# Attention and two MoE layers on one core: the order of exponentials, casts and low parts in the attention stage, and the first forget-gate rows spread by TensorE

## The chip, the cores and the metric

The kernel runs on one NeuronCore of one Trainium2 chip, in one launch. The metric is the device time of an execution in microseconds (us); a smaller one is better.

## The reference, cut to what matters

Attention with a forget gate over 4 batches, 8 heads, 576 positions and a head size of 64, then an MLP with a piecewise quadratic activation, then a top-1 mixture of 8 experts. What is computed ahead of the second layer:

```python
log_f = np.log(np.clip(f, 0.0001, 1.0))
cum = np.cumsum(log_f, axis=-1)
decay = cum[:, :, :, None] - cum[:, :, None, :]
scores = np.where(causal, -1000000000.0, scale * (q @ k.T) + decay)
scores = scores - np.max(scores, axis=-1, keepdims=True)
attn = np.exp(scores)
attn = attn / (np.sum(attn, axis=-1, keepdims=True) + 1e-09)
x = attn @ v            # heads merged to 2304 x 512
h = x @ w_in            # 512 -> 2048
g = np.where(h >= 1, h, np.where(h <= -1, 0.0, (h + 1) ** 2 / 4))
x = g @ w_out
# then: normalised x and expert_emb give logits / tau, one expert of 8 for each
# token, relu(x @ w1[e]) @ w2[e], times the gate
```

Along a row the term cum of the query is constant and drops out in the softmax, so the kernel only needs the row of the keys' cumulative sums, the same on all 64 query rows of a head.

## The kernel before, in words

All products that need more than one pass are made of a high part (rounded to the fp32r type) and a low part (what is left): high times high, high times low, low times high.

**Attention stage.** The 32 heads are 16 pairs; a pair has 9 query blocks of 64 rows. Both heads of a pair stand one above the other on the 128 partitions, so block i of a pair is a tile of 128 rows and 64(i+1) keys. The 144 tiles are steps n, with `tile_of(n)` giving the pair p and the block i. Each engine has one program written out by hand over n, and semaphores tie them together:

- TensorE (lines 1550 on, helpers at 1434 to 1510): `score(n + 4)` makes the scores of a tile in one of three PSUM banks and adds the causal mask (line 1431). The first two blocks of a pair are one f32 product (line 1447), the others three fp32r ones (1450, 1455). `turn(p, k)` (line 1477) transposes the weights of a pair in eight "fills", each a part of a PSUM bank; fill k needs the exponentials up to its block (0 after block 1, 1 after 3, 2 and 3 after 5, 4 and 5 after 7, 6 and 7 after 8), and as three banks are used in turn it waits for the low part of fill k-3, that is `pt_l`. Fill 7 also turns the inverse denominators of the pair before (1485). `head` (1494) multiplies with v. A score tile waits for the minimum three banks back (`minimum_ahead`): block 8 of a pair waits for the minimum of block 6.
- VectorE (lines 1172 to 1223): `masked(n)` (line 1112) reads the scores and the gate row `c8`, writes minus their scaled sum to `pr` and its minimum to `mmin`. `low(p, k)` (1134, 1131 for fill 7) subtracts the high part from the transposed weights. It also inverts denominators (1118, 1124), copies results (1140, 1146, 1150) and, in pairs 7 to 14, makes the low part of a tile of x (`split_x`, 1155). In step n it does `masked(n + 3)` and then the fills of step n-1.
- ScalarE (lines 902 to 923): `exp(n)` (864) is the exponential with its row sum; `high(p, k)` (874) casts a transposed fill to its high part; `copy_early` (880) copies a result. In step n it does `exp(n + 2)` and then the casts of the fills that belong to the block of step n-1; only where that block is 5 are the casts first:

```python
p, i = tile_of(n - 1)
if i != CASTS_FIRST and 0 <= n + 2 < STEPS:
    exp(n + 2)
if 0 <= n - 1 < STEPS:
    for k in fills_of(i):
        high(p, k)
if i == CASTS_FIRST and 0 <= n + 2 < STEPS:
    exp(n + 2)
```

- GpSimd splits k, q and v of later pairs into high and low parts (lines 624, 626, 638, 640, 648, 650) and adds and scales x (691, 693).
- SyncE issues the loads. The cumulative sums `fc`, which lie in the tile `pr`, are written to DRAM (line 470), and come back as a row broadcast over 64 partitions for each head (line 431; for the second head of pair 0 line 854 on ScalarE's queue).

**Opening.** TensorE runs 22 products on the identity (line 1420) before any data is there. f is clipped, its logarithm and its cumulative sum are taken (1077, 846, 1079, 1081). GpSimd zeroes parts of `pr` once `fc` has been stored (661). VectorE normalises the expert embedding (1211 to 1219) before the first `masked`; TensorE turns it (1557) at step 0, ScalarE and VectorE split it at steps 1 and 2 (921, 1222).

**Behind it.** The MLP, with three products for each term (1523 to 1525), and the experts. The attention stage ends at about 200 us of the profile.

Of the kernel before, what the change touches and what calls it, by code (L numbers as in the profile page):

```python
# [5 lines left out]
ALU = mybir.AluOpType  # L6
# [9 lines left out]
P = 128  # L16
# [4 lines left out]
def attention_moe_kernel(nc, q, k, vk, f, w_in, w_out, expert_emb, tau, w1, w2, out):  # L21
# [58 lines left out]
    EARLY = 2  # L80
    CASTS_FIRST = 5

# [24 lines left out]
    with ExitStack() as ctx:  # L107
# [106 lines left out]
        rden = sb("rden", [P, 2, NB], F32, actx)  # L214

        emb, emb_sq, norm_e = xo[0:E, 1, 0, 0:DM], xo[0:E, 1, 1, 0:DM], xo[0:E, 1, 0, DM:DM + 3]

# [50 lines left out]

        f_in = sem("f_in"); clip_ok = sem("clip_ok"); log_ok = sem("log_ok"); cum_ok = sem("cum_ok")
        cum_done = sem("cum_done"); cum_out = sem("cum_out")  # L270
        passed = sem("passed")
# [127 lines left out]
        def _(sp):  # L399
# [26 lines left out]
            def load_c(p):  # L426
                if p >= 2:
                    sp.wait_ge(lowest, NB * (p - 1))

                for h in range(2 if p else 1):  # L430
                    sp.dma_start(c8[h * D:(h + 1) * D, p % 2, :],
                                 cum_d[2 * p + h:2 * p + h + 1, :].to_broadcast([D, S])).then_inc(c_in[p % 2], 16)
# [19 lines left out]
            def load_x(n):  # L452
# [6 lines left out]
                for h in range(2):  # L459
# [10 lines left out]
            sp.dma_start(cum_d, fc).then_inc(cum_out, 16)  # L470
            sp.wait_ge(cum_out, 16)
            load_c(0)
            load_k(1)
            load_v(0)
            sp.dma_start(xst[:].rearrange("p a c -> p (a c)")[:, 0:(NB - RAW) * P],
                         q[1, :, RAW:NB, :].rearrange("p i r -> p (i r)")).then_inc(q1_in, 16)
            load_first(1)
            load_c(1)
            load_k(2)
# [126 lines left out]
        def _(pool):  # L606
# [50 lines left out]
            pool.wait_ge(const_ok, 2)  # L657
            nc.gpsimd.memset(rinv[:], 0.0).then_inc(zero_ok, 1)
            pool.wait_ge(cum_out, 16)
            for i in range(0, NB, 2):  # L660
                x = nc.gpsimd.memset(pr[:, at_tile(i) + keys(i):at_tile(i) + keys(i) + D], 0.0)
# [181 lines left out]
        def _(act):  # L843
# [8 lines left out]
            nc.scalar.copy(qh[:, 0], qraw[:]).then_inc(q_h, 1)  # L852
            act.wait_ge(cum_out, 16)
            act.dma_start(c8[D:P, 0, :], cum_d[1:2, :].to_broadcast([D, S])).then_inc(c_in[0], 16)
            act.wait_ge(esq_ok, 1)
# [46 lines left out]
            for n in range(-AHEAD, STEPS + 1):  # L902

                p, i = tile_of(n - 1)
                if i != CASTS_FIRST and 0 <= n + 2 < STEPS:
                    exp(n + 2)
                if 0 <= n - 1 < STEPS:
                    for k in fills_of(i):
                        high(p, k)
                if i == CASTS_FIRST and 0 <= n + 2 < STEPS:  # L910
                    exp(n + 2)
# [5 lines left out]
                if n == STEPS:  # L917
                    rise(0)
                if n == 1:
                    act.wait_ge(en_turned, 1)  # L920
# [135 lines left out]
        def _(dve):  # L1056
# [35 lines left out]
            def masked(n):  # L1092
                p, i = tile_of(n)
                w = keys(i)
                if i == 0:
                    dve.wait_ge(c_in[p % 2], 32 * (p // 2 + 1))
                if n == 0:
# [74 lines left out]
            for n in range(-AHEAD, STEPS + TAIL):  # L1172
# [7 lines left out]
                if 0 <= n - 1 < STEPS:  # L1180
                    for k in fills_of(i):
                        low(p, k)
                    if i == 8 and p >= 1:
                        copy_turned(p - 1)
# [22 lines left out]
                if n == STEPS + 4:  # L1207
                    add(1)
                    low_g(1)
                if n == -AHEAD:  # L1210
                    step(nc.vector.reciprocal(tau_inv[:], tau_sb[:]))
# [7 lines left out]
                    nc.vector.tensor_scalar(emb, emb, norm_e[:, 1:2], None, ALU.mult).then_inc(en_ok, 1)  # L1219
                if n == 2:  # L1220
                    dve.wait_ge(ent_h, 1)
# [194 lines left out]
        def _(pe):  # L1416
            pe.wait_ge(const_ok, 2)

            for n in range(WARM):
                nc.tensor.matmul(psum[:, PY, :].rearrange("p (a b) -> p a b", a=4), ident_b[:],  # L1420
                                 ident_b[:].unsqueeze(1).to_broadcast([P, 4, P]), start=True, stop=True)


            MASK_LATER = (4,)
# [120 lines left out]
            for n in range(-AHEAD, STEPS + TAIL):  # L1545
# [6 lines left out]
                if n == STEPS - 1:  # L1552
                    up_block(1)
                if n == 0:
                    pe.wait_ge(en_ok, 1)
# [263 lines left out]
```

## Time and profile before

| what | value |
|---|---|
| median of 3 runs | 849.34 us (848.88 to 849.74) |
| the profiled execution's own time | 848.67 us |
| its span, first to last instruction | 846.5 us |
| TensorE busy | 831.4 us, 98% |
| VectorE, ScalarE, GpSimd busy | 410.8, 392.9, 353.0 us |
| mean granted TensorE clock | 0.996 of full speed |

The profile is one execution. Its times count from the first instruction. PE is TensorE, PEld its weight loads, DVE VectorE, ACT ScalarE, POOL GpSimd, SPq the DMA issues of SyncE. TensorE's records overlap each other, since its products are pipelined, so a record's length says less than the distance between starts. A note in square brackets is idle time of that engine just before the instruction and what ended it.

### The profile page before, as it was taken

How to read it: one execution, taken by the hardware profiler on the slowest of the kernel's cores; microseconds unless marked ns; L12 is line 12 of the kernel's file. 1: busy time of each engine (PE TensorE's matmuls, PEld its weight loads, DVE VectorE, ACT ScalarE, POOL GpSimd, SP SyncE). 2: the span in 40 equal slices, each digit the busy share in tenths (PEclk: the TensorE clock that was granted, in tenths of full speed). 3: DMA queues.
4: the chain of work that ended last, by engine and by line, in shares of the span. 5: the costliest groups of instructions: out<-in, count | busy, mean ns of one | idle time of the engine just before them, and what ended most of it. 6: DMA issues, size and time to landing. Idle time of an engine off the chain costs nothing.

```text
span 846.5 us, 13803 instructions
## 1 busy us (share of the span) xinstructions
PE 831.4 (98%) x5018; PEld 778.9 (92%) x5019; DVE 410.8 (49%) x1002; ACT 392.9 (46%) x916; POOL 353.0 (42%) x366
## 2 busy tenths in 40 slices
PE   7999999999999999999999999999999999999996
PEld 5888888889999999999999999999998998998985
DVE  5888888887555454454444444455534110110200
ACT  6777877876665444534544534433332121111121
POOL 5776778856665020211111202074311692010295
PEclk9999999999999999999999999999999999999999
DMA  7577988962000310301211033252222354304041
GB/s 223 189 246 232 288 264 285 291 207 57 29 1 2 102 57 29 104 29 56 75 56 57 1 103 106 75 163 63 76 101 87 120 167 125 87 37 125 26 138 42
DMA packets 70941, 95.62 MB, mean 113 GB/s; under 512 B 7174, under 2 KB 47110, under 8 KB 70864
## 3 DMA queue, kind: packets, MB, share of 16 engines
q1 hardware_dynamic: 62688, 80.33, 31.3%
q10 hardware_dynamic: 6416, 9.59, 3.2%
q0 software_dynamic: 1760, 4.72, 1.5%
q8 instruction: 43, 0.70, 0.3%
q14 instruction: 34, 0.28, 0.1%
HBM read 70.87 MB, written 24.27 MB: 112 GB/s over the span
## 4 chain that ended last, share of the span: by engine, by line
PE 96%; DVE 2%; DMA 1%; issue 1%; ACT 0%; POOL 0%; POOLq 0%; DVEq 0%; SPq 0%; ACTq 0%
PE psum L1523 25%; PE psum L1525 24%; PE psum L1524 24%; PE psum L1494 6%; PE psum L1450 5%; PE psum L1477 5%; PE psum L1455 2%; PE psum L1447 1%; PE psum L1431 1%; DVE pr L1112 1%; PE psum L1606 1%; PE psum L1590 0%; PE psum L1591 0%; DMA c<-cum_d 0%; DVE ptl L1134 0%
## 5 line engine op out<-in xcount | busy, mean ns | idle before, releaser
L1523 PE MATMUL psum<-xh,winh 128*128 128x384 f32 x384 | 129.0, 336 | 0.0
L1523 PE MATMUL psum<-gh,wouth 128*128 128x384 f32 x384 | 128.3, 334 | 0.2 <-issue 0.2
L1525 PE MATMUL psum<-xh,winl 128*128 128x384 f32 x384 | 128.4, 334 | 0.0
L1524 PE MATMUL psum<-xl,winh 128*128 128x384 f32 x384 | 128.3, 334 | 0.0
L1525 PE MATMUL psum<-gh,woutl 128*128 128x384 f32 x384 | 128.3, 334 | 0.0
L1524 PE MATMUL psum<-gl,wouth 128*128 128x384 f32 x384 | 128.3, 334 | 0.0
L898 ACT ACTIVATE hpos<-psum,minus 128x384 f32<-128x384 f32 x96 | 55.9, 582 | 142.3 <-DVE hclip L1160 142.1
L1165 DVE TENSOR_TENSOR g<-hpos,hsq 128x384 f32<-128x384 f32 x96 | 64.5, 672 | 109.2 <-ACT hsq L900 109.2
L691 POOL TENSOR_TENSOR xst<-xst 128x384 f32<-128x384 f32 x24 | 24.7, 1031 | 178.4 <-DMA xst<-rinv_d 178.2
L1270 DVE SCALAR_TENSOR_TENSOR hl<-psum,hh 128x384 fp32r<-128x384 f32 x48 | 26.8, 558 | 139.4 <-ACT hh L954 139.4
L1169 DVE TENSOR_TENSOR gl<-g,gh 128x384 fp32r<-128x384 f32 x96 | 64.1, 668 | 61.0 <-ACT gh L931 61.0
L864 ACT ACTIVATE pr<-pr,mmin 128x64 f32<-128x64 f32 (+2 forms) x144 | 81.3, 568 | 24.3 <-DVE mmin L1112 24.1
L931 ACT CAST gh<-g 128x384 fp32r<-128x384 f32 x96 | 49.4, 514 | 75.7 <-DVE g L1165 75.7
L1134 DVE TENSOR_TENSOR ptl<-psum,pth 128x512 fp32r<-128x512 f32 (+1 forms) x112 | 65.8, 611 | 22.8 <-ACT pth L874 22.6
L1112 DVE CUSTOM_DVE_ANT_0 pr<-psum,c 128x64 f32<-128x64 f32 (+2 forms) x144 | 67.8, 476 | 10.0 <-PE psum L1431 8.7
L1523 PEld LDWEIGHTS psum<-xh,winh 128*128 128x128 f32 x384 | 72.1, 188 | 0.4
L1523 PEld LDWEIGHTS psum<-gh,wouth 128*128 128x128 f32 x384 | 72.1, 188 | 0.5 <-issue 0.5
L1524 PEld LDWEIGHTS psum<-xl,winh 128*128 128x128 f32 x384 | 72.1, 188 | 0.0
L1525 PEld LDWEIGHTS psum<-xh,winl 128*128 128x128 f32 x384 | 72.1, 188 | 0.0
L1525 PEld LDWEIGHTS psum<-gh,woutl 128*128 128x128 f32 x384 | 72.1, 188 | 0.0
L1524 PEld LDWEIGHTS psum<-gl,wouth 128*128 128x128 f32 x384 | 72.1, 188 | 0.0
L1160 DVE TENSOR_SCALAR hclip<-psum 128x384 f32<-128x384 f32 x96 | 53.0, 552 | 28.4 <-PE psum L1525 28.2
(233 smaller groups left out, 1871.6 us busy)
## 6 DMA issues: line engine op xcount, KB each, us to landing
praw<-moe_w SPq DMA_DIRECT2D x48, 256.0 KB, 2.8
qraw<-q SPq DMA_DIRECT2D x15, 448.0 KB, 4.5
vraw<-vk SPq DMA_DIRECT2D x16, 320.0 KB, 3.8
xh<-yh_d SPq DMA_DIRECT2D x20, 256.0 KB, 4.2
xl<-yl_d SPq DMA_DIRECT2D x20, 256.0 KB, 4.6
kraw<-k SPq DMA_DIRECT2D x16, 288.0 KB, 3.8
xa_d<-xo SPq DMA_DIRECT2D x16, 288.0 KB, 4.0
xb_d<-xo SPq DMA_DIRECT2D x16, 288.0 KB, 4.5
```

The lines of the kernel that those rows point to most:

```text
L864: nc.scalar.activation(region, region, ACT.Exp, bias=mmin[:, p % 2, i:i + 1], scale=-1.0, accum_out=rsum[:, p % 2, i:i + 1]).then_inc(expe ...
L898: nc.scalar.activation(hpos[:], psum[:, UP[u % 2], 0:CH], ACT.Relu, bias=minus[:, 0:1]).then_inc(up_read, 1)
L931: nc.scalar.copy(gh[:, u % NG, :], g[:]).then_inc(g_h, 1)
L1112: nc.vector.tensor_tensor_reduce(out=out_at, in0=src, in1=c_at, scale=-SCALE, scalar=LARGE, op0=ALU.add, op1=ALU.min, accum_out=mmin[:, p ...
L1134: nc.vector.tensor_tensor(stacked(ptl, k), of_bank(p, k), stacked(pth, k).bitcast(F32), ALU.subtract).then_inc(pt_l, 1)
L1160: nc.vector.tensor_scalar(hclip[:], psum[:, UP[u % 2], 0:CH], -1.0, 1.0, ALU.max, ALU.min).then_inc(clipped, 1)
L1165: nc.vector.tensor_tensor(g[:], hpos[:], hsq[:], ALU.add).then_inc(summed, 1)
L1169: nc.vector.tensor_tensor(gl[:, u % NG, :], g[:], gh[:, u % NG, :].bitcast(F32), ALU.subtract).then_inc(g_l, 1)
L1494: x = nc.tensor.matmul(dst[:, (i - i0) * D:ni * D], vv[:, p % 2, b, h, :], src, start=n == 0, stop=n == len(todo) - 1)
L1523: nc.tensor.matmul(psum_at, ah, bh, start=start, stop=False)
L1524: nc.tensor.matmul(psum_at, ah, bl, start=False, stop=False)
L1525: return nc.tensor.matmul(psum_at, al, bh, start=False, stop=stop)
```

## The change

1. In the attention stage ScalarE does the casts before the exponential also where the block of step n-1 is 7 or 8 (fills 4 and 5 before the exponential of block 1 of the next pair, fills 6 and 7 before that of block 2).
2. VectorE makes the low part of fill 0 a step later, behind `masked` of block 6 where it stood behind that of block 5.
3. The gate rows of pair 0 no longer go through DRAM: GpSimd makes a 2 x 128 matrix of ones and zeros (`spread`), TensorE multiplies it with `fc` of heads 0 and 1 (two f32 products of 288 columns, behind the 22 products on the identity and before the first scores), and ScalarE copies the result from PSUM to `c8`. GpSimd's zeroing of `pr`, where `fc` lies, waits for these products too. The two broadcast loads of pair 0 go away; SyncE waits for the stored sums only before pair 1's gate rows, behind the loads of k, v, q and the first blocks of pair 1.
4. The embedding's normalisation moves from VectorE's first step (n = -4) to n = 0, behind `masked(3)`; its transposes from n = 0 to 3, ScalarE's copy from 1 to 4, VectorE's low part from 2 to 5.

```diff
-    CASTS_FIRST = 5
+    CASTS_FIRST = (5, 7, 8)
...
+        spread = rturn[0:2, 0, :]
...
             def load_c(p):
                 if p >= 2:
                     sp.wait_ge(lowest, NB * (p - 1))
-
-                for h in range(2 if p else 1):
+                for h in range(2):
...
             sp.wait_ge(cum_ok, 1)
             sp.dma_start(cum_d, fc).then_inc(cum_out, 16)
-            sp.wait_ge(cum_out, 16)
-            load_c(0)
             load_k(1)
             load_v(0)
...
             load_first(1)
+            sp.wait_ge(cum_out, 16)
             load_c(1)
...
             nc.gpsimd.memset(rinv[:], 0.0).then_inc(zero_ok, 1)
+            nc.gpsimd.memset(spread, 1.0).then_inc(spread_ok, 1)
+            pool.wait_ge(spread_ok, 1)
+            nc.gpsimd.affine_select(out=spread, in_=spread, compare_op=ALU.is_ge, fill=0.0, base=0,
+                                    pattern=[[1, P]], channel_multiplier=-D).then_inc(spread_ok, 1)
+            pool.wait_ge(spread_ok, 2)
+            nc.gpsimd.affine_select(out=spread, in_=spread, compare_op=ALU.is_ge, fill=0.0, base=D - 1,
+                                    pattern=[[-1, P]], channel_multiplier=D).then_inc(spread_ok, 1)
             pool.wait_ge(cum_out, 16)
+            pool.wait_ge(c_spread, 1)
...
-            act.wait_ge(cum_out, 16)
-            act.dma_start(c8[D:P, 0, :], cum_d[1:2, :].to_broadcast([D, S])).then_inc(c_in[0], 16)
+            act.wait_ge(c_spread, 1)
+            nc.scalar.copy(c8[:, 0, :].rearrange("p (a c) -> p a c", a=2), psum[:, PX:PY + 1, 0:S // 2]).then_inc(c_first, 1)
             act.wait_ge(esq_ok, 1)
...
-                if i != CASTS_FIRST and 0 <= n + 2 < STEPS:
+                if i not in CASTS_FIRST and 0 <= n + 2 < STEPS:
                     exp(n + 2)
...
-                if i == CASTS_FIRST and 0 <= n + 2 < STEPS:
+                if i in CASTS_FIRST and 0 <= n + 2 < STEPS:
                     exp(n + 2)
...
-                if n == 1:
+                if n == 4:
                     act.wait_ge(en_turned, 1)
...
-                if i == 0:
-                    dve.wait_ge(c_in[p % 2], 32 * (p // 2 + 1))
+                if n == 0:
+                    dve.wait_ge(c_first, 1)
+                elif i == 0:
+                    dve.wait_ge(c_in[p % 2], 32 * ((p + 1) // 2))
...
-                    for k in fills_of(i):
+
+                    for k in fills_of(i) if i not in (1, 2) else fills_of(i - 1):
                         low(p, k)
...
-                if n == -AHEAD:
+                if n == 0:
                     step(nc.vector.reciprocal(tau_inv[:], tau_sb[:]))
...
-                if n == 2:
+                if n == 5:
                     dve.wait_ge(ent_h, 1)
...
+            pe.wait_ge(cum_ok, 1)
+            pe.wait_ge(spread_ok, 3)
+            for j in range(2):
+                x = nc.tensor.matmul(psum[:, PX + j, 0:S // 2], spread, fc[0:2, j * (S // 2):(j + 1) * (S // 2)],
+                                     start=True, stop=True)
+            x.then_inc(c_spread, 1)
...
-                if n == 0:
+                if n == 3:
                     pe.wait_ge(en_ok, 1)
```

## Rows read from the trace of the kernel before

**Rows 1.** The page, the chain that ended last: shares of the span by engine.

```profile
PE 96%; DVE 2%; DMA 1%; issue 1%; ACT 0%; POOL 0%; POOLq 0%; DVEq 0%; SPq 0%; ACTq 0%
```

**Rows 2.** Busy time by stretch, behind the attention stage; each engine's busy us (instructions).

```profile
400.00:600.00 200.00, 200.00 (x1162) 197.19 (x1162) 99.66 (x184) 86.62 (x172) 53.57 (x51) 1.00 0.23 74
```

**Rows 3.** Timeline: TensorE's transposes of fills 6 and 7, pairs 0, 3, 4.

```profile
23.20 0.74 PE L1477 MATMUL psum<-ident,pr 128*128 128x128 f32 x5
...
58.30 0.30 PE L1477 MATMUL psum<-ident,pr 128*128 128x128 f32 x1
...
69.11 1.05 PE L1477 MATMUL psum<-ident,pr 128*128 128x128 f32 x5
```

**Rows 4.** Timeline of pair 4: what leads to fill 7 on the three engines.

```profile
67.34 1.07 PE L1477 MATMUL psum<-ident,pr 128*128 128x128 f32 x8
...
68.03 0.40 ACT L864 ACTIVATE pr<-pr,mmin 128x128 f32<-128x128 f32 x1
...
68.41 1.06 ACT L874 CAST pth<-psum 128x512 fp32r<-128x512 f32 x2
...
69.02 1.29 DVE L1134 TENSOR_TENSOR ptl<-psum,pth 128x512 fp32r<-128x512 f32 x2 [0.70 <-ACT pth L874]
```

**Rows 5.** Timeline of pair 4: low part of fill 0, minimum of block 6, scores of 8.

```profile
62.06 0.42 DVE L1134 TENSOR_TENSOR ptl<-psum,pth 128x256 fp32r<-128x256 f32 x1 [0.50 <-ACT pth L874]
...
62.40 0.61 DVE L1112 CUSTOM_DVE_ANT_0 pr<-psum,c 128x448 f32<-128x448 f32 x1
...
63.08 0.40 PE L1455 MATMUL psum<-kh,qh 128*128 128x288 f32 x1
```

**Rows 6.** Who waited for whom; line 1155 (min/median/max ns); timeline of pair 8.

```profile
PE psum L1455 <- DVE mmin L1112: 0.8, 3, 0.4
...
L1155 DVE TENSOR_TENSOR xl<-xst,xh x8: 540/577/1121, 95.7 to 177.2; 128x384 fp32r<-128x384 f32 x8
...
106.85 0.95 POOL L638 TENSOR_SCALAR qh<-qraw 128x896 fp32r<-128x896 f32 x1
...
107.25 0.94 DVE L1155 TENSOR_TENSOR xl<-xst,xh 128x384 fp32r<-128x384 f32 x1
```

**Rows 7.** Timeline: the denominators of pair 1, of pair 4 beside them.

```profile
32.77 1.55 POOL L650 TENSOR_TENSOR vv<-vraw,vv 128x640 fp32r<-128x640 f32 x1
...
32.92 1.43 DVE L1118 TENSOR_SCALAR rden<-rsum 128x9 f32<-128x9 f32 x1
...
35.37 0.30 PE L1477 MATMUL psum<-ident,pr 128*128 128x128 f32 x1 [0.54 <-DVE ptl L1134]
...
67.83 0.18 DVE L1118 TENSOR_SCALAR rden<-rsum 128x9 f32<-128x9 f32 x1
```

**Rows 8.** The opening: timeline, and a stretch with PEclk third from the end.

```profile
8.64 1.28 ACT L864 ACT_TABLE_LOAD   x1
...
9.69 0.47 PE L1447 MATMUL psum<-kf,qf 128*128 128x128 f32 x2
...
9.97 0.47 DVE L1219 TENSOR_SCALAR xo<-xo 8x512 f32<-8x512 f32 x1
...
11.73 0.23 DVE L1112 CUSTOM_DVE_ANT_0 pr<-psum,c 128x64 f32<-128x64 f32 x1 [1.29 <-DMA c<-cum_d]
...
12.02 0.39 PE L1450 MATMUL psum<-kh,qh 128*128 128x256 f32 x1 [1.39 <-DVE mmin L1112]
...
12.54 0.68 POOL L624 TENSOR_SCALAR kh<-kraw 128x576 fp32r<-128x576 f32 x1 [4.16 <-DMA kraw<-k]
...
14.91 0.49 DVE L1112 CUSTOM_DVE_ANT_0 pr<-psum,c 128x320 f32<-128x320 f32 x1 [1.76 <-PE psum L1431]
...
18.04 2.12 POOL L640 TENSOR_TENSOR ql<-xst,qh 128x896 fp32r<-128x896 f32 x1
...
20.19 0.49 PE L1447 MATMUL psum<-kf,qf 128*128 128x128 f32 x2 [0.26 <-DVE mmin L1112]
...
14.00:16.00 2.00, 2.00 (x10) 1.57 (x8) 0.98 (x4) 0.55 (x2) 1.92 (x3) 0.50 0.90 220
```

More of the change, by code:

```diff
@@ L269, in attention_moe_kernel @@
         f_in = sem("f_in"); clip_ok = sem("clip_ok"); log_ok = sem("log_ok"); cum_ok = sem("cum_ok")
+        spread_ok = sem("spread_ok"); c_spread = sem("c_spread"); c_first = sem("c_first")
         cum_done = sem("cum_done"); cum_out = sem("cum_out")
```

## The prediction

> **What bounds the kernel now.** I read the page first, then busy time by stretch, then the timeline of TensorE pair by pair, looking for places where it stands still. The chain that ended last is TensorE for 96% of the span [rows 1]. Behind the attention stage TensorE never rests: 200.00 us busy of 200.00 [rows 2]. So a microsecond gained or lost before 200 us should reach the end whole, and one gained on another engine counts only where TensorE waits for it. The reader should look for three kinds of wait.
>
> A small one that returns. In fills 6 and 7 TensorE makes five transposes. In pair 0 they take 0.74 us, in pair 4 1.05 us, and all that makes the difference is a stop before the fifth, the one of fill 7; pairs 2 to 14, thirteen in all, show the same 1.04 or 1.05 [rows 3]. Of the 0.31 us, 0.03 is that the last record itself is longer after a stop (0.30 for 0.27), so the stop costs about 0.28 us. The view of waits doesn't list it, since the records overlap.
>
> One that comes now and then: the scores of block 8 wait for the minimum of block 6 three times, 0.8 us in all [rows 6], in pairs 8, 9 and 14.
>
> And the opening with pair 1: TensorE is idle 1.39 us at 12.02, when the gate row has come through DRAM and VectorE has stood 1.29 us for it; it waits again at 20.19 and, for 0.54, at 35.37 [rows 7, 8].
>
> **Casts first at blocks 7 and 8.** Fill 7 waits for the low part of fill 4. In pair 4 that starts at 69.02, after VectorE has stood 0.70 us for ScalarE's cast; the cast starts at 68.41, after the exponential of the next pair's block 1, at 68.03 [rows 4]. Fill 4 is the first half of eight transposes that start at 67.34: its last one starts three distances of 0.11 later and takes 0.27, so it is ready at about 67.97. With the order turned round, the cast starts at 68.03, 0.38 earlier, and the low part starts at 68.64 and ends, 0.69 later, at 69.33. Counting the 0.15 us that TensorE needs after the old end (69.71, next transpose at about 69.86), fill 7 may start at 69.48. TensorE gets there at 69.58. The stop goes, with 0.10 to spare: 13 x 0.28 = 3.6 us. The bounds are 0 and 13 x 0.31 = 4.0.
>
> What is late in exchange: the exponential of block 1 by the two casts, 1.06 - 0.1 us [rows 4], that of block 2 by two more. ScalarE's total is the same, so the exponential of block 3 isn't moved. Fill 0, which needs block 1's, comes about 1.5 us after its new end; that is the cover, and I cost this at nothing. Without it, up to 1 us a pair would appear before fill 0.
>
> **Low part of fill 0 behind block 6's minimum.** VectorE now stands 0.50 us for the cast, works 0.42, and only then makes the minimum at 62.40, which ends at 63.0; TensorE asks for it at 63.08 [rows 5]. So in an ordinary pair it comes by a hair, and the order gains nothing there. In pairs 7 to 14 `split_x` stands before it as well: 0.54 us when undisturbed, 0.94 in pair 8, where GpSimd's cast at 106.85 was running when it came, 1.12 at most [rows 6]. The three pairs whose `split_x` took longest are those where TensorE waited. Afterwards the minimum of block 6 follows block 5's at once; with the 0.17 us that VectorE gains on TensorE from the earlier casts, an undisturbed `split_x` leaves 0.5 to 0.6 us of room. The disturbances of 0.4 to 0.6 us are then just covered. I take 0.7 of the 0.8 us; bounds -0.5 (a longer disturbance) and 1.1 (with the 0.09 that records overlap at each). The low part of fill 0 itself is needed by fill 3, some 3 us later: nothing. Without that move, the first part would run into this wait in every pair, since it takes 0.28 from TensorE's way and leaves the minimum where it is.
>
> **The opening.** TensorE's identity products end at about 9.5. An f32 product of 128 columns is two records in 0.47 us with a pipeline's tail of 0.27, so some 0.11 for each pass [rows 8]; 288 columns in two passes, twice, is 4 x 0.25 = 1.0 us. The spread is in PSUM at about 10.6. GpSimd's zeroing ends near 11.15. ScalarE's copy of 576 columns is about 0.7 us (two casts of 512 take 1.06 in sequence [rows 4]): 11.35. The first minimum starts at 11.4 for 11.73, and the scores of block 3 at 11.7 for 12.02: 0.3 us, with 1.0 us of TensorE's new work inside what was idle. ScalarE's exp table, loaded at 8.64 in idle time, now loads behind copy and root, from 11.55 to 12.85 [rows 8], and the first exponential starts 0.85 later; the first fill, at 14.7 before, needs block 1's by then, which comes at 13.7: hidden.
>
> Two things gain more. TensorE's clock was at half, 0.50, from 14 to 16 us [rows 8], after the stop of 1.39 us; with only some tenths idle there it may stay at 2.4 GHz. And VectorE needn't wait for fill 0 before the minimum of block 6. One thing takes: the normalisation of the embedding, 8.76 to 10.44 in idle time before (its last operation starts at 9.97 [rows 8]), now stands between the minima of blocks 3 and 4, about 12.8 to 14.5. The minimum of block 4 started at 14.91 after 1.76 us of idling, so undisturbed it fits. By these steps the first wait of pair 1 ends at about 19.1 for 20.19: a gain of 1.1 us.
>
> But GpSimd is no longer idle there. Its split of pair 1's k, which waited 4.16 us for a load until 12.54 [rows 8], starts about 1.4 us earlier, at 11.15, its load being issued before the gate rows. The row on denominators shows what that can do: 128x9 numbers took 1.43 us, to the end of GpSimd's 1.55 us subtraction, and 0.18 otherwise [rows 7]. The last operation of the normalisation, 8x512, arrives at about 14.0, between GpSimd's cast of v and its subtraction of 1.55 us. If it comes first it loses 0.1, if second up to 1.5; if all four such operations of the chain are held up like this, the minimum of block 4 starts at about 17.3, and pair 1 1.5 us later than before. So the opening is worth from -1.5 to 1.6 us. I take 0.6, between the free and the once-blocked case.
>
> By the Trainium skill (SBUF — State Buffer, section "Who interferes with whom") VectorE's two-port modes and its operations on two SBUF operands take a port pair that GpSimd shares, and the later one waits for the whole instruction. By that rule, the trace agrees: 1.43 for 0.18 us. It speaks against moving the normalisation: by it the opening would be worth about 0, and -1.5 if the one-element operations count too, which no row shows.
>
> **Pair 1.** The same hold-up cost TensorE 0.54 us before fill 7, 0.7 by the distance of starts [rows 7]. GpSimd's chain moves by 1.4 us and TensorE by 0.6, so the subtraction ends some 0.8 us earlier against the denominators: I take 0.6, bounds 0 and 0.7. If the opening gains more, this gains less.
>
> **Sum.** 3.6 + 0.7 + 0.6 + 0.6 = 5.5 us. The profiled execution would take 848.67 - 5.5 = 843.2 (span 841.0). It stands 0.67 below the median of the runs, so the median goes to 849.34 - 5.5 = 843.8. All removed and the opening at its best gives 4.0 + 1.1 + 1.6 + 0.2 = 6.9, or 842.4.
>
> **Rivals.**
> (a) *The opening backfires*, every operation of the chain held up: -1.5 there, 0.7 in pair 1, the rest as said: 849.34 - 3.5 = 845.8. For it: GpSimd works without a break from 11 to 19 us. Against it: only operations of many elements are seen held up.
> (b) *The small stop stays or another takes its place*: the room of 0.10 us is thin, and if the cast waits for the transposes rather than for the exponential, fill 7 stops as before. 849.34 - 1.9 = 847.4; half of it, 845.6. Against: the cast followed the exponential's end without a gap.
> (c) *The change does nothing that counts*: the opening's gain and loss cancel and (b) holds: about 849.3.
> (d) *Slower*: VectorE reaches `split_x` earlier and meets GpSimd's longest operation, 2.12 us [rows 8], in all of pairs 7 to 14. Beyond the room of 0.55 that is 1.57 us x 8 = 12.6: 849.34 - 5.5 + 12.6 = 856.4. It decides from a mean hold-up of 0.55 + 5.5/8 = 1.2 us. Against it: of eight, none was held up over 0.6, and the shift between the two engines is 0.17 us.
>
> **How the numbers follow.** About 0.2% (1.7 us) is what a measurement of this kernel can tell from no change. My forecast has 0.68, (a) 0.14, (b) 0.10, (c) 0.05, (d) 0.03. Faster by over 0.2%, below 847.6: forecast, (a) and most of (b), less something for what I haven't seen, 0.90. Within: 0.06. Slower: 0.04. The range reaches from the best sum, widened by 0.4 for the spread of runs (848.88 to 849.74), 842.0, to beyond (a), 846.3.
>
> **What would show it.** Right: five transposes of fills 6 and 7 in 0.74 us in all pairs, VectorE's idling of 0.70 before the low part of fill 4 shorter by about 0.4; no wait of line 1455 for a minimum; the minimum of block 6 right behind block 5's; the first minimum at 11.4; a full clock from 13 to 17 us. Wrong: line 1219 or 1215 with more than a microsecond, the minimum of block 4 after 15 us; five transposes still in 1.05; `split_x` above 1.2 us; a new wait of TensorE before fill 0 for an exponential; a gap behind 200 us that was not there.

## The result, and the profile after the change

The changed kernel took 840.87 us (median of 4 runs, 840.24 to 841.81), the kernel before beside it 849.54 (848.88 to 850.49): a ratio of 0.9898, 95% interval 0.9881 to 0.9915. The gain is 8.7 us where 5.5 was predicted, and 840.87 lies 1.1 us below the low end of the range. The profiled execution took 840.24 us with a span of 838.1.

The page of the changed kernel, the chain that ended last and TensorE's busy time; then its busy time by stretch, behind the attention stage and in the opening:

```profile
PE 98%; DVE 1%; issue 1%; ACT 0%; POOL 0%; POOLq 0%; ACTq 0%
...
PE 826.5 (99%) x5022; PEld 778.4 (93%) x5023; DVE 412.8 (49%) x1002; ACT 393.1 (47%) x917; POOL 353.7 (42%) x369
```

```profile
400.00:600.00 200.00, 200.00 (x1162) 197.19 (x1161) 100.79 (x184) 86.11 (x172) 57.61 (x55) 1.00 0.25 77
```

TensorE has 98% of the chain for 96 [rows 1] and is as full as before behind the attention stage [rows 2]. So all of the gain must lie ahead of the first product with `winh`. It does; the timelines of TensorE, before and after:

```profile
194.92 0.39 PE L1523 MATMUL psum<-xh,winh 128*128 128x384 f32 x1
```

```profile
186.58 0.39 PE L1543 MATMUL psum<-xh,winh 128*128 128x384 f32 x1
```

From there to the end it is 846.5 - 194.92 = 651.6 us before and 838.1 - 186.58 = 651.5 after: the shift of 8.34 us reaches the end whole.

**A table that settles most of it.** The records of TensorE overlap, so a stop of a tenth isn't in the view of waits. Starts don't overlap. I took from the timelines the start s(p) of the 192-column scores of block 2 in every pair p. Here are the profiled executions of both kernels and of the 16 experiment kernels, in us; "later" is s(3) to s(15), twelve pairs:

```
kernel                            s(0)   s(1)   s(1)-s(2)  s(2)-s(3)  later    s(15) to winh
before                           10.02  21.04     10.98      11.81    139.75      11.35
changed                          11.12  19.74     10.98      11.81    133.30      10.75
e1 casts only                    10.11  20.10     10.98      11.12    135.33      10.90
e2 low part of fill 0 only        9.98  20.68     10.98      11.63    137.39      11.06
e3 both orders, old opening      10.38  20.13     11.00      11.07    133.25      10.75
e4 new opening only              11.38  20.52     11.35      11.55    140.72      11.34
e5 casts of 7, not 8             11.96  20.57     11.30      11.52    138.11      10.99
e6 casts of 8, not 7             11.82  20.43     10.98      11.83    136.55      11.05
e7 denominators later            12.34  20.96     11.27      11.07    135.51      10.76
e8 chain first                   11.75  19.77     10.98      11.07    133.61      10.76
e9 spread in warm-up             12.73  25.79     12.31      11.07    134.33      11.35
e10 both of these                13.08  20.76     10.98      11.07    133.83      10.76
e11 changed again                12.29  20.92     10.98      11.78    133.50      10.75
e12 as e3, again                 10.31  20.14     11.00      11.07    134.03      10.76
e13 18 identity products         10.42  19.04     10.98      11.78    133.90      10.75
e14 18 products, chain first     10.09  18.53     10.98      11.07    133.51      10.75
e15 as e8, again                 11.87  19.89     10.98      11.07    134.40      10.75
e16 changed, third               11.03  19.65     10.98      11.84    134.63      10.75
```

Between before and changed the 8.34 us are: 1.30 up to s(1); nothing in s(1) to s(3), which holds the stop of pair 1 (11.81 with it, 11.07 to 11.12 without: e1, e3, e12 and six more kernels have lost it); 6.45 in the twelve later pairs; 0.60 behind s(15). An ordinary pair takes 11.55 us before and 11.07 to 11.08 after, 0.475 less. Twelve of them are 5.7; the other 0.75 is what the longer pairs gave back: three took 11.84 to 12.01 us before, and after the longest takes 11.39. The table holds one execution of each kernel; where it ranks kernels, the medians below decide.

**Where 0.475 comes from.** Fill 7, as predicted. The transposes of fills 6 and 7 in pair 4, changed kernel, with ScalarE and VectorE beside them:

```profile
66.72 0.42 ACT L874 ACTIVATE pr<-pr,mmin 128x128 f32<-128x128 f32 x1
...
66.86 0.74 PE L1497 MATMUL psum<-ident,pr 128*128 128x128 f32 x5
```

```profile
65.77 1.07 ACT L884 CAST pth<-psum 128x512 fp32r<-128x512 f32 x2
...
66.39 1.29 DVE L1146 TENSOR_TENSOR ptl<-psum,pth 128x512 fp32r<-128x512 f32 x2 [0.32 <-ACT pth L884]
```

The cast of fill 4 now stands ahead of the exponential, VectorE stands 0.32 us for it and not 0.70, and five transposes take 0.74 for 1.05 [rows 3, 4]. Pairs 0 and 2 to 14 all show 0.74, but for one with 0.88, where the denominators before it were held for 0.84 us. By starts the stop was worth 0.30 (e6, below, has it back and takes 11.38 a pair).

The other 0.17 is a stop that I had called none. TensorE from fill 1 to the scores of block 8, first before, then changed:

```profile
62.54 0.63 PE L1477 MATMUL psum<-ident,pr 128*128 128x128 f32 x4
...
63.32 0.30 PE L1455 MATMUL psum<-kl,qh 128*128 128x288 f32 x1
```

```profile
60.46 0.64 PE L1497 MATMUL psum<-ident,pr 128*128 128x128 f32 x4
60.85 0.38 PE L1475 MATMUL psum<-kh,qh 128*128 128x288 f32 x1
61.06 0.30 PE L1475 MATMUL psum<-kl,qh 128*128 128x288 f32 x1
```

From the first transpose to the first scores it is 63.08 - 62.54 = 0.54 us before [rows 5] and 0.39 after, and from there to the next product 0.24 and 0.21. Before, pairs 0 to 2 have the short distance as well and pairs 3 to 15, thirteen, the long one. The records of the transposes are as long in both, so nothing of it shows in a duration.

**The opening.** Timeline of the changed kernel, all engines (answers to [rows 8]):

```profile
9.33 1.23 PE L1439 MATMUL psum<-pr,rturn 2*128 2x288 f32 x4
...
10.60 0.64 ACT L864 COPY c<-psum 128x576 f32<-128x576 f32 x1 [2.97 <-PE psum L1439]
...
11.33 0.22 DVE L1124 CUSTOM_DVE_ANT_0 pr<-psum,c 128x64 f32<-128x64 f32 x1 [2.58 <-PE psum L1451]
11.92 1.43 POOL L628 TENSOR_TENSOR kl<-kraw,kh 128x576 fp32r<-128x576 f32 x1
...
12.86 0.14 DVE L1226 TENSOR_SCALAR xo<-xo 8x1 f32<-8x1 f32 x1
...
13.22 0.26 DVE L1228 TENSOR_SCALAR xo<-xo 8x1 f32<-8x1 f32 x1
...
13.88 0.47 DVE L1232 TENSOR_SCALAR xo<-xo 8x512 f32<-8x512 f32 x1
...
14.12 1.66 POOL L652 TENSOR_TENSOR vv<-vraw,vv 128x640 fp32r<-128x640 f32 x1
...
14.28 0.47 DVE L1124 CUSTOM_DVE_ANT_0 pr<-psum,c 128x320 f32<-128x320 f32 x1
...
18.89 0.49 PE L1467 MATMUL psum<-kf,qf 128*128 128x128 f32 x2 [0.26 <-DVE mmin L1124]
```

The first minimum starts at 11.33 (11.4 predicted); two small operations of the chain start at 12.86 and 13.22, inside GpSimd's subtraction of 11.92 (it ends at 13.35), and take 0.14 and 0.26 as in the kernel before, so they aren't held; the large one comes 0.24 us ahead of the next subtraction and isn't either. The first wait of pair 1 ends at 18.89 for 20.19. TensorE's clock is full here, where it was at half before:

```profile
14.00:16.00 2.00, 1.86 (x12) 1.23 (x11) 2.00 (x8) 1.61 (x6) 1.92 (x3) 1.00 0.89 251
```

**Pair 1.** Its stop stays, to the hundredth of a microsecond [rows 7]:

```profile
31.46 1.56 POOL L652 TENSOR_TENSOR vv<-vraw,vv 128x640 fp32r<-128x640 f32 x1
...
31.62 1.43 DVE L1130 TENSOR_SCALAR rden<-rsum 128x9 f32<-128x9 f32 x1
...
34.07 0.30 PE L1497 MATMUL psum<-ident,pr 128*128 128x128 f32 x1 [0.54 <-DVE ptl L1146]
```

### The profile page after: what moved, and what is told of

Its sections match the earlier page's. It is cut to its first block, busy times and chain, and to the rows that moved or that the text cites. A ratio compares the mean times of both kernels' runs of the same rounds, so it can differ in the third digit from the quotient of the medians.

```text
span 838.1 us, 13816 instructions
## 1 busy us (share of the span) xinstructions
PE 826.5 (99%) x5022; PEld 778.4 (93%) x5023; DVE 412.8 (49%) x1002; ACT 393.1 (47%) x917; POOL 353.7 (42%) x369
## 4 chain that ended last, share of the span: by engine, by line
PE 98%; DVE 1%; issue 1%; ACT 0%; POOL 0%; POOLq 0%; ACTq 0%
PE psum L1543 25%; PE psum L1544 25%; PE psum L1545 25%; PE psum L1514 6%; PE psum L1470 6%; PE psum L1497 5%; PE psum L1475 1%; PE psum L1467 1%; PE psum L1433 1%; PE psum L1451 1%; PE psum L1626 1%; PE psum L1610 1%; PE psum L1611 0%; DVE ptl L1146 0%; ACT pr L874 0%
## 5 line engine op out<-in xcount | busy, mean ns | idle before, releaser
L884 ACT CAST pth<-psum 128x512 fp32r<-128x512 f32 (+2 forms) x128 | 57.8, 494 | 22.2 <-PE psum L1497 21.6
```

The costliest lines, as they stand in the source:

```text
L884: nc.scalar.copy(stacked(pth, k)[0:rows], of_bank(p, k)[0:rows]).then_inc(pt_h, 1)
```

## The experiments

My theory after the two traces was that the two orders carry the gain by removing both stops of an ordinary pair; the rivals stand in each expectation.

**One part at a time.** e1 takes the casts alone, e2 the low part of fill 0 alone, e3 both; the opening is that of before in all three.

```
e1, e3:  CASTS_FIRST = (5, 7, 8)
e2, e3:  for k in fills_of(i) if i not in (1, 2) else fills_of(i - 1):
             low(p, k)
```

> The kernel before with the casts first also at blocks 7 and 8, nothing else. Theory A (TensorE stood about 0.17 us before the scores of block 8 in every pair, waiting for the minimum of block 6, and that minimum hangs on the casts too): the stop before fill 7 goes (0.30 us a pair, 13 pairs) and, since VectorE's whole sequence comes 0.45 us earlier, so does most of the one before block 8: a pair takes about 11.1 us for 11.55, and the time falls by about 6 us, to 843.5. Theory B (only the order of the low part of fill 0 removes the stop before block 8): the gain is 0.30 x 13 = 4 us at most, less what comes back before block 8, so 845.5 to 848, and the distance from the last transpose of fill 1 to the scores of block 8 grows to 0.3 us.

> The kernel before with the low part of fill 0 behind block 6's minimum, nothing else. Both theories keep the stop before fill 7. Theory A: 0.17 us in each of 14 pairs and the 0.8 us of the three long waits go: about 3.2 us, 846.3. My recorded step (an ordinary pair gains nothing): 0.7 us, 848.8.

> The kernel before with both orders, the opening as it was. Theory A: a pair takes 11.08 us and the gain is 6.2 us in the pairs and 0.8 in the three long waits, about 7: 842.5; hardly more than the casts alone. Theory B: the sum of the two parts alone.

Measured: e1 842.59 us (841.63 to 843.25; ratio 0.9923, 0.9906 to 0.9940), e2 845.22 (844.78 to 845.48; 0.9952, 0.9935 to 0.9968), e3 840.05 (839.89 to 843.28; 0.9905, 0.9881 to 0.9929). The orders alone give the whole gain. The split that I expected was off: e3 gains 2.5 us more than e1, where I had said hardly more. In the traces e3's first product with `winh` comes 8.7 us sooner where 7 was expected; the rest is 0.9 us before s(1) and 0.7 at pair 1, whose stop is gone. e2 leaves fill 7's stop and takes 0.17 from every ordinary pair (11.38). The same two transposes-and-scores of pair 4 in e2, then in e1:

```profile
61.82 0.64 PE L1477 MATMUL psum<-ident,pr 128*128 128x128 f32 x4
62.21 0.38 PE L1455 MATMUL psum<-kh,qh 128*128 128x288 f32 x1
```

```profile
60.16 0.63 PE L1477 MATMUL psum<-ident,pr 128*128 128x128 f32 x4
60.59 0.40 PE L1455 MATMUL psum<-kh,qh 128*128 128x288 f32 x1
```

0.39 us in e2. In e1 it is 0.43, and its ordinary pairs take 11.12 to 11.13: the casts alone bring the minimum of block 6 forward against TensorE and remove all but 0.05 of both stops. I had said that the first part without the second would run into this wait in every pair; it runs into 0.05 of it. What e1 lacks is room for `split_x`: its scores of block 8 wait three times, 1.1 us in all, and its later pairs take 135.33 for 133.25 in e3. There the second part earns its place.

**The opening alone** (e4: the changed kernel with both orders undone).

> The changed kernel with the casts and the low part of fill 0 in the old order: only the spread gate rows and the later embedding. If the opening is worth what the first wait of pair 1 says (it ends at 18.9 for 20.2), 1.3 us: 848.2; the three minima that had not to wait for fill 0 come from the other order, so without it some of that is lost: 0.5 to 1.3 us. Granted clock between 13 and 17 us full if the stop of 1.39 us was its cause.

Measured 849.66 us (848.57 to 850.82; ratio 1.0003, 0.9993 to 1.0014): no gain where 0.5 to 1.3 us was expected. s(1) comes 0.52 us sooner, and the later pairs take 0.97 more. Who waited for whom, e4:

```profile
PE psum L1475 <- DVE mmin L1124: 1.4, 7, 0.2
```

Seven waits for the minimum of block 6 where before had three [rows 6]. `split_x` took 0.94 to 0.96 us in seven of the eight pairs, by its timeline: with the old order each such hold-up reaches TensorE, and seven pairs take 11.83 to 11.87 for 11.56. In this trace the opening's gain is lost where the two engines now meet; that another execution would meet in the same way isn't shown.

**The casts apart** (e5 and e6: the changed kernel with one block left out).

```
e5:  CASTS_FIRST = (5, 7)
e6:  CASTS_FIRST = (5, 8)
```

> The changed kernel with the casts first at block 7 but no longer at block 8. If the stop before fill 7 hangs on the cast of fill 4 alone, and the minimum of block 6 has room enough by the order of fill 0, pairs stay at 11.07 us and the time at about 841. If the earlier casts of fills 6 and 7 are what pays for the minimum, a pair takes 11.1 to 11.25 us and the time is 841.5 to 843.5.

> The changed kernel with the casts first at block 8 but no longer at block 7. The stop of 0.30 us before fill 7 comes back in pairs 2 to 14: a pair takes 11.38 us, the time is 841 + 4 = 845. If it stays near 841, the cast of fill 4 was not held by the exponential but by the transposes.

Measured: e5 844.60 us (843.77 to 845.86; ratio 0.9942, 0.9925 to 0.9958), e6 844.68 (844.23 to 845.54; 0.9949, 0.9933 to 0.9966). e6 has fill 7's stop back and pairs of 11.38: right. e5 is a miss (841 to 843.5 expected): it has lost that stop, but its ordinary pairs take 11.31 and not 11.07. Pair 4 of e5:

```profile
68.20 0.74 PE L1497 MATMUL psum<-ident,pr 128*128 128x128 f32 x5
...
69.37 0.73 ACT L884 CAST pth<-psum 128x512 fp32r<-128x512 f32 x2
...
70.00 0.69 DVE L1146 TENSOR_TENSOR ptl<-psum,pth 128x512 fp32r<-128x512 f32 x1 [0.57 <-ACT pth L884]
...
70.72 0.28 DVE L1143 TENSOR_TENSOR pth<-psum,pth 64x128 fp32r<-64x128 f32 x1
...
70.79 0.20 PE L1451 MATMUL psum<-mask_b,ident_b 128*128 128x64 bf16 x1
...
71.06 0.85 PE L1514 MATMUL psum<-pth,vv 128*128 128x320 f32 x5
```

The transposes are done sooner, and the next thing to be late is the attention product that needs fills 6 and 7: it starts 0.27 us behind the mask product, when VectorE's part of fill 7 is made (70.72 and 0.28). In the changed kernel the cast of fill 6 stands ahead of the exponential too (67.58 us for 69.37, as against the transposes 0.72 behind their start and not 1.17), and no such gap is left. So the casts of block 8 don't remove a stop of before; they remove the one that block 7's alone would bring. I had foreseen neither. Seven of e5's eight `split_x` took 0.94 to 1.46 us as well, and its pairs from 8 to 14 are longer still, 11.51 to 12.02, so the 0.24 isn't all of the 3.7 us that e5 loses.

**Pair 1's stop** (e7 puts the denominators one block later).

```
-                if i == 7 and 0 <= p < PAIRS:
-                    denominator(p)
                 if i == 8 and 0 <= p < PAIRS:
+                    denominator(p)
                     invert(p)
```

> The changed kernel with the denominators' sum (the 128x9 TENSOR_SCALAR) a step later, behind the low parts of fills 4 and 5, right before their inverse. If GpSimd's subtraction of v held VectorE up there in pair 1, the stop of 0.70 us before fill 7 of pair 1 goes, and with it 0.7 us: 840.2. If the stop has another cause (the loads of pair 2), it stays and so does 840.9.

Measured 843.00 us (842.17 to 843.31; ratio 0.9924, 0.9908 to 0.9941): a miss. Pair 1 is rid of its 0.7, but from pair 7 on the operation meets GpSimd at its new place (timeline of e7, `rden` in one of the later pairs):

```profile
147.20 0.98 DVE L1130 TENSOR_SCALAR rden<-rsum 128x9 f32<-128x9 f32 x1
```

It ends at 148.18, with GpSimd's operation on `xst` that ran from 147.14 for 1.02 us. TensorE stands for the next minimum, that pair takes 11.73 for 11.07, and the later pairs take 135.51 in all.

**The chain of the normalisation ahead of the first minima** (e8): its operations go back to where they stood before the change, and ScalarE's square root goes ahead of its copy.

```
-            act.wait_ge(c_spread, 1)
-            nc.scalar.copy(c8[:, 0, :]...).then_inc(c_first, 1)
             act.wait_ge(esq_ok, 1)
             nc.scalar.activation(norm_e[:, 1:2], norm_e[:, 0:1], ACT.Sqrt).then_inc(eroot_ok, 1)
+            act.wait_ge(c_spread, 1)
+            nc.scalar.copy(c8[:, 0, :]...).then_inc(c_first, 1)
...
-                if n == 0:
+                if n == -AHEAD:
                     step(nc.vector.reciprocal(tau_inv[:], tau_sb[:]))
```

> The changed kernel with the embedding's root ahead of ScalarE's copy of the gate rows and its normalisation back in VectorE's idle time before the first minimum (8.8 to 10.5 us), the transposes and splits left where the change put them. If the normalisation behind the minimum of block 3 is what delays the opening now (the minimum of block 4 starts at 14.28, the masked scores are there at about 13.35), that minimum starts 0.8 us earlier, the exp table loads in idle time as well, and the first wait of pair 1 ends about 0.8 us earlier, at 18.1: 840.1. If the opening hangs on the casts and low parts of fills 1 to 3, nothing or 0.2 us.

Measured 839.84 us (839.30 to 840.64; ratio 0.9890, 0.9873 to 0.9906), where 840.1 was expected. s(0) to s(1) takes 8.01 for 8.62, and pair 1 has no stop: GpSimd's cast of v waits there for its load and came at 31.33 us for 30.65, so that the denominators met the cast and not the subtraction. The new opening isn't needed for that. In e3, with both orders and the opening of before:

```profile
31.97 0.73 POOL L648 TENSOR_SCALAR vv<-vraw 128x640 fp32r<-128x640 f32 x1 [3.12 <-DMA vraw<-vk]
32.03 0.69 DVE L1118 TENSOR_SCALAR rden<-rsum 128x9 f32<-128x9 f32 x1
```

There too they met the cast, were held for half a microsecond and not 1.25, and pair 1 lost its stop.

**Is the opening worth anything, and what does it stand behind?** In the table the openings of the changed kernel (changed, e11, e16) reach s(1) at 19.74, 20.92 and 19.65: 1.3 us apart for one kernel. Their spread starts right behind the identity products. e11, TensorE:

```profile
7.60 2.97 PE L1433 MATMUL psum<-ident_b 128*128 128x512 bf16 x11
10.50 1.23 PE L1439 MATMUL psum<-pr,rturn 2*128 2x288 f32 x4
```

10.50 us for 9.33 in the profiled run above: the 22 products were busy 7.6 us for 6.5. From start to start they first stand 0.43 us apart and then 0.22. The slower pace lasts for seven distances in the changed kernel's trace and in e16's and for thirteen in e11's; six more at 0.21 us each account for the difference. e9 puts the spread behind 8 identity products, with 10 more after it (18 in all, written to another PSUM bank, since the spread's result stands in the old one); e10 does so in e8 (where its expectation says the denominators' chain, the normalisation's is meant); e11 and e12 repeat the changed kernel and e3.

```
e9, e10:
+            warm(8)
             pe.wait_ge(cum_ok, 1)
...
+            warm(10)
```

> The changed kernel with its spread of the first gates no longer behind all 22 identity products but between 8 of them and 10 more. Theory A (the changed opening now follows the end of the identity products, which differs by up to 2 us from run to run): the spread is there near 8 us, the copy near 9, the first minimum before 10.5 us for 11.33, and the scores of block 2 of pair 0 start before 11 us whatever the identity products take; the chain of fill 0 then sets pair 1, so that the start of the scores of pair 1 comes 0 to 1 us earlier: 840.0 us. Rival B (the opening's time is given back in later pairs whatever it gives): within 0.3 us of the changed kernel. Rival C: fewer identity products ahead of the first scores leave TensorE at half clock for longer, 842 us.

> The kernel with the denominators' chain ahead of the first minima, and the spread between 8 and 10 identity products as well. Theory A: the scores of block 2 of pair 0 start before 11 us and the chain no longer delays the minimum of block 4, so that the scores of pair 1 start near 19 us for 19.77: 839.0 us. Rival B (given back later): 839.8, as with the chain moved alone. Rival C (half clock for longer): 841.

> The changed kernel once more, beside the others of this call: 840.9 us as before by every theory; it gives the reference on the same chip.

> Both orders (casts of blocks 5, 7 and 8 first, the low part of fill 0 behind the minimum of block 6) with the opening of before, once more beside the changed kernel. Theory A (the new opening is worth nothing in the total): within 0.4 us of the changed kernel of this call, 840.3 to 841.3. Rival B (it is worth what the first wait of pair 1 showed, 1.3 us, less what pair 1 gives back, 0.7): the kernel with the opening of before is 0.6 us slower, 841.5.

Measured: e9 844.44 us (840.23 to 848.53; ratio 0.9935, 0.9911 to 0.9959), e10 841.00 (838.66 to 841.93; 0.9896, 0.9879 to 0.9913), e11 840.97 (840.56 to 841.54; 0.9902), e12 840.58 (840.29 to 840.65; 0.9898). e11 and e12 ran side by side: the new opening isn't worth anything in the total, and with e3 and e16 it looks 0.4 us or more slower. The table says where: the changed kernel has s(1) 0.4 us ahead of e3 and e12 (19.74 for 20.13 and 20.14) and then the stop of pair 1, 0.74, which they have lost; its s(3) is at 42.53 for 42.20 and 42.21.

One thing speaks for the new opening. The mean granted clock of an execution was 0.997 or more in all thirteen runs of changed, e11 and e16 and in e4's ten, but in only 23 of 40 runs of the kernel before. Its other 17 took 849.9 us on the average for 848.7. Of the eight runs of e3 and e12 one has the lower clock, 0.994, and it is the slow one, 843.28. The profiled executions of before and e2, with half the clock in the opening, have 0.996 each. So the new opening spares the kernel these executions and is slower than the others: e4's 849.66 is to be set beside 848.7.

e9 and e10 miss. Their four spread products fall into the slower pace, between identity products that still stand 0.43 us apart: they take 722 ns each for 427 behind all 22, and s(0) comes later than ever. But e9's slowest run, the profiled one, shows what my rival (a) was about. VectorE, GpSimd and TensorE of e9:

```profile
15.41 2.45 DVE L1232 TENSOR_SCALAR xo<-xo 8x512 f32<-8x512 f32 x1
17.80 0.47 DVE L1124 CUSTOM_DVE_ANT_0 pr<-psum,c 128x320 f32<-128x320 f32 x1
```

```profile
15.38 2.08 POOL L642 TENSOR_TENSOR ql<-xst,qh 128x896 fp32r<-128x896 f32 x1
```

```profile
18.33 0.79 PE L1472 MATMUL psum<-kh,qh 128*128 128x512 f32 x1 [2.50 <-DVE mmin L1124]
```

```profile
20.00:22.00 2.00, 2.00 (x11) 1.65 (x11) 1.09 (x3) 1.48 (x5) 0.00 (x0) 0.50 0.00 0
```

The last operation of the chain came 0.03 us behind GpSimd's longest one and took 2.45 us for 0.47. TensorE stood 2.50 us for the minimum behind it, then ran at half clock, and s(1) comes at 25.79. Six runs of e9 took 840.23, 842.36, 842.44, 846.43, 846.76 and 848.53 us, with a mean granted clock of 0.998, 0.996, 0.996, 0.994, 0.994 and 0.995. So the clock was lower in all five slow ones; only the slowest was profiled, so that the same meeting was behind the others is argued, not shown.

**Fewer identity products** (e13 in the changed kernel, e14 in e8; `WARM = 18` for 22), with e8 and the changed kernel once more beside them (e15, e16).

> The changed kernel with 18 identity products ahead of the spread instead of 22. Theory A (the new opening stands behind the end of the identity products): the spread starts 4 products of 0.21 to 0.43 us sooner, 0.9 to 1.7 us, and the scores of pair 1 start as much sooner, 18.5 to 19.5 us, if the chain of the normalisation meets no long operation of GpSimd; pair 1 keeps or loses its stop of 0.7: 840.0 us. Rival B (the normalisation's last operation, then nearer to GpSimd's long ones, is held 1.5 to 2 us as in the ninth run): scores of pair 1 at 21 us or later, 841.5 us or more. Rival C (given back later): as the changed kernel.

> The chain ahead of the first minima and 18 identity products. Theory A: the scores of pair 1 start at 18.5 to 19 us for 19.77, nothing can be held in the opening, 839.0 us. Rival C (given back later by hold-ups in pairs 7 to 14): 839.8.

> The chain ahead of the first minima, once more beside the changed kernel. Theory A: 0.5 to 1.1 us below it (no stop of 0.7 in pair 1, the minimum of block 4 sooner): 840.0 us where the changed kernel takes 840.9. Rival: no difference beyond 0.3 us.

> The changed kernel as the reference of this call: 840.9 us by every theory.

Measured: e13 840.23 us (839.85 to 840.59; ratio 0.9896, 0.9881 to 0.9911), e14 839.52 (838.37 to 839.91; 0.9888, 0.9873 to 0.9903), e15 839.89 (838.78 to 840.60; 0.9886, 0.9871 to 0.9901), e16 841.35 (840.70 to 842.47; 0.9908, 0.9894 to 0.9921). The spread starts at 8.62 and 8.30 us in e13 and e14, s(1) comes at 19.04 and 18.53. e14, VectorE's chain and first minimum:

```profile
10.35 0.73 DVE L1232 TENSOR_SCALAR xo<-xo 8x512 f32<-8x512 f32 x1
11.01 0.20 DVE L1124 CUSTOM_DVE_ANT_0 pr<-psum,c 128x64 f32<-128x64 f32 x1
```

The 8x512 operation was held a little even here (0.73 for 0.47 us), where I had expected none to be. Theory A was right in direction: e13 and e15 lie 1.1 and 1.5 us below e16, which ran beside them, and e14, with both, 1.8 us below it, with ranges that don't touch (e13's by only 0.1 us, and it overlaps with the earlier runs of the changed kernel). e14 beats both the changed kernel and the one before; beyond e15 it isn't told apart (0.4 us, ranges overlapping). In the profiled runs pair 1's stop is there in each of changed, e6, e11, e13 and e16, in part in e5, and in none of e8, e10, e14 and e15: with the chain first it goes. With the opening of before it is there in before and e2, the two with half the clock, and not in e1, e3 and e12.

## Why the prediction was wrong in size

The direction, the engine and the two places were right, and TensorE's shift reached the end whole. By its terms, against the 8.34 us of the two traces:

- **Fill 7, 3.6 us.** Right: 0.30 by starts for the 0.28 used, in thirteen pairs, 3.9. The bounds (0 to 4.0) held. The reason was right as well: cast at once behind block 1's exponential of the next pair before, ahead of it now.
- **Low part of fill 0, 0.7 us: the step that failed.** "So in an ordinary pair it comes by a hair, and the order gains nothing there." It didn't come by a hair, it came late, by 0.17 us in each of pairs 3 to 15: 2.2 us over thirteen, which the sum put at nothing. The prediction took 63.08, when the scores started, for when TensorE asked for the minimum. By its own 0.11 for a transpose, four of them from 62.54 let the scores start at 62.98; the changed kernel's 0.39 for 0.54 and e2, with this part alone, show that they can start earlier still. The low end of the range left the term out too: "all removed" with it is 6.9 + 2.2 = 9.1, or 840.2 us. The longer pairs gave 0.75 (1.15 us over the ordinary ones in all before, 0.40 after), where 0.7 was taken.
- **"Without that move, the first part would run into this wait in every pair."** Wrong for the ordinary pairs: e1 pays 0.05 us in each. The casts move VectorE's minimum forward along with TensorE; I had left it where it is. Right for three of the pairs with `split_x`, where e1 still waits 1.1 us.
- **The casts late in exchange, nothing.** The exponentials were covered, as said. But I asked only for what the exponentials delay and not for who needs fills 6 and 7 next: e5 shows 0.24 us a pair there, which the casts of block 8 take away again. The sum was saved by a part of the change whose purpose I hadn't seen.
- **The opening, 0.6 us.** The trace gives 1.30 up to pair 1, inside the range of -1.5 to 1.6, and step by step (11.33, clock, chain at 14.3) as reckoned. But with the opening of before and both orders, e3 and e12 reach s(1) at 20.13 and 20.14: 0.9 of the 1.30 comes without the new opening. They have the full clock without it, and the execution of before that I had read was one with half the clock. The rest, 0.4, is less than the 1.3 by which the new one differs between executions, and e4 gained nothing in the total. So the term's 0.6 is not a gain of the new opening; that the two traces agree with it is luck. The error was to take one execution's opening, its clock and the end of its identity products at 9.5 us, as the kernel's.
- **Pair 1, 0.6 us.** It was 0. I let GpSimd's chain move by 1.4 and TensorE by 0.6. GpSimd's v waits for its load (2.96 us of idling ahead of its cast), and subtraction and denominators both moved by 1.3: 32.77 to 31.46 and 32.92 to 31.62 [rows 7]. In e3 they moved apart, and the stop's 0.74 was gained.

Sum: 3.9 + 2.2 + 0.75 + 1.30 + 0 = 8.15, and the remaining 0.2 lies behind s(15), where the last pair shows 0.60 for the two stops' 0.475, and in rounding.

**The rivals.** (a) didn't come true: the operations of one element weren't held. By the Trainium skill (SBUF — State Buffer, section "Who interferes with whom") a VectorE instruction in a two-port mode and a GpSimd instruction take turns, and the later one waits for the whole of the other. The trace of e9 agrees for the operation of 8x512, 2.45 for 0.47 us. Those of 8x1 weren't held in the changed kernel; whether they run in such a mode no run shows. The rule speaks against the place of the chain, and rightly: in the changed kernel the long hold-up was missed by 0.24 us. (b), a small stop in place of another, is what e5 is. (c) fell. (d) fell for the changed kernel: its longest `split_x` is 1.27 us, once, in the pair of 11.39, where the denominators were held too. In e4, without the room, it was real in small: seven times 0.29 us, 0.97 more than before, where three pairs were long already.

Open remains why TensorE's pace doubles after seven identity products in one run (6.5 us for the 22) and after thirteen in another (7.7).

## What to carry to other kernels

When TensorE is nearly always busy, measure it by distances from start to start, pair against pair and against the sum of undisturbed distances: a stop of 0.17 us that recurs thirteen times is in no view of waits, and was a quarter of the result. When a stop is taken away, ask who reads each of the moved results next, not only what was pushed back. And a local gain in an opening counts only beside the same kernel with the old opening: an end that wanders by a microsecond from run to run can't be read from one trace. Look further than the first place where the gain shows, too: here 0.4 us was won before pair 1 and 0.74 lost in it.

## What the runs showed of the hardware

What a hold-up between VectorE and GpSimd costs depends on hundredths. The same 8x512 operation took 0.47 us when it came 0.24 us ahead of a GpSimd subtraction, and 2.45 when it came 0.03 us behind one of 2.08 us. `rden` took 0.16 to 0.19 us free and up to 2.10 held (e9), `split_x` 0.54 free and up to 1.66.

TensorE's granted clock in the opening fell to half, 1.2 GHz, in the executions where TensorE had stood for 1.39 us (before), 1.07 (e2) and 2.50 (e9), and stayed at 2.4 GHz where it had stood for 0.94 (e1), 0.65 (e3) and 0.73 us (e12). The stretch from 13 to 17 us (granted clock third from the end), first e2, then e3:

```profile
13.00:17.00 4.00, 4.00 (x18) 2.86 (x16) 2.02 (x8) 2.29 (x9) 3.92 (x4) 0.57 0.89 265
```

```profile
13.00:17.00 4.00, 4.00 (x31) 3.21 (x31) 2.56 (x10) 2.98 (x11) 3.83 (x5) 1.00 0.84 260
```

The opening of before had a better clock in e1, e3 and e12 for reasons that aren't in the changed orders, since those come into play only behind the stop. In e1, e2, e3 and e12 the first minimum started at 11.35 to 11.37 us for 11.73 in before, and in e3 and e12 the identity products ended at 10.02 and 9.95 us for 9.66, so that TensorE came to the stop later.

The identity products ran at two paces in every trace, 0.43 us from start to start and then 0.22; where there are 22, seven to thirteen distances are at the slower one. The granted clock reads 1.00 from 2 to 6 us in all traces, so it doesn't show this.
